# Retention and two MLPs on one core: the key-value product of a head pair as two 64x64 products on the diagonal

## The reference

```python
state = np.zeros((B, H, D, D))                 # B=4, H=8, S=768, D=64
for t in range(S):
    state = gamma[None, :, None, None] * state + np.einsum('bhd,bhe->bhde', k[:, :, t], v[:, :, t])
    y[:, :, t] = scale * np.einsum('bhd,bhde->bhe', q[:, :, t], state)
```

## Time and profile before

| | before |
|---|---|
| median of 3 runs | 1049.16 us (1048.57 to 1049.89) |
| span of the profiled execution | 1048.8 us |
| TensorE matmul busy | 1023.9 us (98%) |
| VectorE busy | 460.4 us (44%) |
| ScalarE busy | 431.9 us (41%) |
| GpSimd busy | 90.4 us (9%) |
| mean granted TensorE clock | 0.995 |

### The profile page before, as it was taken

One profiled execution on the slowest core, in us unless ns is written; L12 is line 12 of the kernel. 1 busy time (PEld: TensorE's weight loads), 2 busy tenths in 40 slices (PEclk: granted clock), 3 DMA queues, 4 the chain that ended last, 5 costly groups with the idle time before them and its releaser, 6 DMA issues.

```text
span 1048.8 us, 15480 instructions
## 1 busy us (share of the span) xinstructions
PE 1023.9 (98%) x5496; PEld 900.6 (86%) x5496; DVE 460.4 (44%) x874; ACT 431.9 (41%) x776; POOL 90.4 (9%) x101
## 2 busy tenths in 40 slices
PE   6799999999998999999999999999999999999998
PEld 4489999999998999999999888888888888888886
DVE  3847635356352463433324653253253254244243
ACT  3445333243231442413223464364364264265255
POOL 5321110111001011100000000000000000000000
PEclk9999999999999999999999999999999999999999
DMA  7664331532314234313134403013012012012000
GB/s 229 210 217 146 106 108 52 166 114 93 119 46 138 98 113 136 111 51 120 66 115 135 137 21 101 1 60 100 0 60 90 10 60 90 10 60 91 11 21 31
DMA packets 75656, 95.51 MB, mean 91 GB/s; under 512 B 7248, under 2 KB 59728, under 8 KB 75600
## 3 DMA queue, kind: packets, MB, share of 16 engines
q1 hardware_dynamic: 71856, 81.11, 24.1%
q0 software_dynamic: 3744, 13.63, 3.9%
HBM read 64.04 MB, written 30.67 MB: 90 GB/s over the span
## 4 chain that ended last, share of the span: by engine, by line
PE 93%; DVE 2%; DMA 1%; ACT 1%; issue 1%; SPq 0%; POOL 0%; DVEq 0%; ACTq 0%; POOLq 0%
PE psum L284 28%; PE psum L286 28%; PE psum L285 27%; PE psum L521 3%; PE psum L531 3%; PE psum L609 2%; PE psum L513 1%; DMA w_raw<-weights 1%; PE psum L548 1%; DMA v_buf<-v_rows 0%; PE psum L501 0%; DVE w_gv_lo L936 0%; ACT L802 0%; DMA chunk_decay_t<-chunk_decay 0%; DVE probs L897 0%
## 5 line engine op out<-in xcount | busy, mean ns | idle before, releaser
L284 PE MATMUL psum<-xn_hi,w_gv_hi 128*128 128x384 f32 x768 | 267.1, 348 | 1.0 <-issue 1.0
L286 PE MATMUL psum<-xn_hi,w_gv_lo 128*128 128x384 f32 x768 | 258.4, 336 | 2.6 <-issue 2.6
L285 PE MATMUL psum<-xn_lo,w_gv_hi 128*128 128x384 f32 x768 | 257.7, 336 | 0.0
L764 ACT ACTIVATE silu<-psum 128x384 f32<-128x384 f32 x96 | 47.2, 492 | 283.6 <-PE psum L286 283.6
L284 PEld LDWEIGHTS psum<-xn_hi,w_gv_hi 128*128 128x128 f32 x768 | 145.2, 189 | 4.3 <-issue 3.4
L286 PEld LDWEIGHTS psum<-xn_hi,w_gv_lo 128*128 128x128 f32 x768 | 144.9, 189 | 2.9 <-issue 2.9
L285 PEld LDWEIGHTS psum<-xn_lo,w_gv_hi 128*128 128x128 f32 x768 | 145.3, 189 | 0.9
L998 DVE TENSOR_TENSOR act_buf<-psum,silu 128x384 f32<-128x384 f32 x96 | 53.5, 557 | 199.9 <-PE psum L286 116.7
L284 PE MATMUL psum<-act_hi,w_out_hi 128*128 128x512 f32 x288 | 114.2, 397 | 0.0
L286 PE MATMUL psum<-act_hi,w_out_lo 128*128 128x512 f32 x288 | 112.3, 390 | 0.0
L285 PE MATMUL psum<-act_lo,w_out_hi 128*128 128x512 f32 x288 | 112.3, 390 | 0.0
(11 more groups left out here) (82 smaller groups left out, 1453.2 us busy)
## 6 DMA issues: line engine op xcount, KB each, us to landing
act_dram<-act_buf SPq DMA_DIRECT2D x96, 192.0 KB, 1.8
act_raw<-act_dram SPq DMA_DIRECT2D x72, 256.0 KB, 2.8
w_raw<-weights POOLq DMA_DIRECT2D x26, 512.0 KB, 4.9
kq_buf<-k_t SPq DMA_DIRECT2D x32, 192.0 KB, 2.8
kq_buf<-q_t SPq DMA_DIRECT2D x64, 96.0 KB, 2.9
k_buf<-k_rows SPq DMA_DIRECT2D x32, 192.0 KB, 2.9
v_buf<-v_rows SPq DMA_DIRECT2D x32, 192.0 KB, 3.1
out<-out_buf SPq DMA_DIRECT2D x24, 256.0 KB, 2.0
```

The lines of the kernel that those rows point to most:

```text
L284: pe.matmul(dst, w_hi, m_hi, start=start, stop=False)
L285: pe.matmul(dst, w_hi, m_lo, start=False, stop=False)
L286: return pe.matmul(dst, w_lo, m_hi, start=False, stop=stop)
L764: act.activation(silu[:, f % 2, :], psum[:, GATE[f % 2], 0:TB], ACT.Silu).then_inc(silu_ready, 1)
```

## The change

The product of decayed keys and values is made as two products, one for each head: 64 stationary columns (the head's decayed keys) against 64 moving columns (the head's values), written to the block on the diagonal that belongs to the head. The two blocks off the diagonal aren't computed any more; nobody read them. The semaphore is incremented by the second product. Nothing else changes.

```diff
                 at_least(pe, state_ready, 2 * (b * BKV + states_before(ch)))
-                pe.matmul(psum[:, KV, 0:P], k_dec[:, r % 2, i, :],
-                          v_buf[:, q, i * P:(i + 1) * P], start=True, stop=True).then_inc(kv_done, 1)
+                for h in range(2):
+                    span = slice(h * HD, (h + 1) * HD)
+                    mm = pe.matmul(psum[span, KV, span], k_dec[:, r % 2, i, span],
+                                   v_buf[:, q, i * P + h * HD:i * P + (h + 1) * HD], start=True, stop=True)
+                mm.then_inc(kv_done, 1)
```

## The result

| | before | after |
|---|---|---|
| median of 5 runs | 1048.57 us (1047.48 to 1049.89) | 1041.79 us (1037.13 to 1042.33) |
| ratio | | 0.9913, 95% interval 0.9888 to 0.9939 |
| span of the profiled execution | 1048.8 us | 1040.0 us |

What follows compares the result with a forecast made beforehand. TensorE, busy 1023.9 of 1048.8 us, was taken as the bound. 1048.8 - 7.0 (products) - 0.4 (half clock) + 0.1 (slack) = 1041.5 us of span, plus 0.36 to the median: 1041.9 us, range 1039.5 to 1046.0.

Steps and rivals of the forecast that it cites:

- Product before, 0.22 us: Retention steps on TensorE: the old two-pass product delays the outputs by 0.22 us, 0.43 with it against 0.21 without.
- The charge for the change of form: TensorE switching from 128*128 to 128*64 matmuls: about 0.09 us, moved ahead of the product and still paid once.
- Two heads side by side, a pass of 0.055, load and stream overlapped: New product on TensorE: two passes delay the outputs by 0.11 us, saving 0.11 to 0.12, taken as 0.115.
- 61 products on the path, slack of 0.1: Of 80 products, 61 at full clock save 0.115 us each, 7.0 in all; VectorE's split keys take back 0.1.
- The product at 74.6 us: Not on the path: TensorE waits 0.6 us for VectorE's split keys behind it, so shortening it only lengthens a wait.
- 0.4 us at half clock in the start: Two products on the path, at 20.5 and 49.3 us, save 0.2 us each at half clock.
- What the program's length may do: 320 more executed instructions may change the gaps and clock at the loop's jump; counted as no change, 1.7 us either way.
- the two gaps: TensorE's waits called issue, 1.0 and 2.6 us, where the loop starts over at 323 us; half clock follows for 3.4 us.
- Rival 1: New passes run one behind the other or load and stream don't overlap: 0.22 us as now, 1049 us; chance 0.09.
- rival 2: TensorE can't be fed the eight instructions per product, limiting from 0.055 us per matmul: up to 1058 us; chance 0.06.
- rival 3: Steps get shorter but waits for VectorE take back 19 of 61 products' gain: 5.1 us saved, 1044 us; chance 0.05.
- its milder estimate of 1.6 us: At about 62 ns of sequencer per matmul a product costs 248 ns: kernel some 1.6 us slower, 1050.8 us.

Runs made afterwards that it cites:

- twice_b: Changed kernel with each pair of narrow products made twice; one execution 1044.3 us, 0.608 us from last scores to the outputs' second pair.
- one_half: Changed kernel with both narrow products on the same half of the array's columns, second head's outputs wrong; median 1042.4 us, ratio 0.9906.
- pad_before: Kernel before the change with 40 more do-nothing semaphore instructions between the gate matmuls of batch 0; 1047.26 against 1051.87 us, ratio 0.995.
- rest_only: Kernel before the change, given the narrow products in batches 1 to 3 only, old product in batch 0; median 1039.44 us, ratio 0.9876.

## Why the prediction was right, and where it was wrong

- **Product before, 0.22 us, read from steps with and without it.** Right: doubling it costs 0.223.
- **The charge for the change of form moves and isn't paid twice.** Right: 0.21 from scores to the new matmuls, none between these and the outputs.
- **Two heads side by side, a pass of 0.055, load and stream overlapped.** Right: 0.107 saved per step (forecast 0.11 to 0.12), and 0.01 more in the gate matmuls behind it, which I hadn't foreseen; on one half of the array it is lost, with twice the width it is lost, doubled it costs 0.116.
- **61 products on the path, slack of 0.1.** About right in sum: 60 products behind 65 us gave 6.9 us; 61 x 0.115 was 7.0. Measured from the gate matmul ahead of a step to the one behind it, 55 of the 60 steps are 0.10 to 0.11 us shorter. The product at 74.6 us is hidden as I said: TensorE's next wait for the split keys is longer by what it saved. TensorE's scores matmul behind it, before and after:

```profile
78.23 0.36 PE L284 MATMUL psum<-kq_hi 128*128 128x256 f32 x1 [0.57 <-DVE kq_lo L904]
80.55 0.35 PE L284 MATMUL psum<-kq_hi 128*128 128x256 f32 x1 [0.68 <-DVE kq_lo L907]
```

  The slack runs out at 120 us (0.09 lost) and at 253 and 391 us (0.03 each), 0.15 where I took off 0.1, and at 85.7 us, which I had missed (0.13).
- **0.4 us at half clock in the start.** Not resolved: the start varies by 6 us with the clock.
- **What the program's length may do.** This is the step that failed. I saw the two gaps and the half clock behind them, wrote that they may shrink, counted no change, and allowed 1.7 us for the clock alone. The term that I put at nothing measured 4.35 us: 2.6 of gap and 1.7 of clock. The change's 160 instructions ahead of the loop moved its head from 6 instructions before the end of a piece to 102. The gap's place, two matmuls behind the head, and the count of added instructions were both at hand, and such a gap, which needs the head in the last 40 or so of 256 instructions, is likelier to go than to stay when the code moves.
- **Rivals.** Rival 1 is refuted by the steps, rival 2 by twice_b (0.035 us a matmul; its milder estimate of 1.6 us should read 61 x 0.028 = 1.7), rival 3 by the stretches (from 65 us to the head they gave 4.5 us for 40 products).
- **The time.** 1041.9 met 1041.79 by luck: in the profiled executions the head's 4.35 us stood against a slow start of 1.9 + 0.4, so a product term that was right met two omissions of opposite sign. With the start as before, the first trace would have ended at about 1037.7 us of span.

## What to carry to other kernels

Before counting an edit that changes the number of instructions ahead of a loop, look at the gaps called issue behind the loop's jump. If one follows the first within a few instructions, the head may lie at the end of a code piece, and then most insertions, useful or not, take the gap away (40, 80, 160, 208 and 480 instructions did here; 256 brought it back); a padding of do-nothing instructions tests that at once. Two 64-column products on different halves of TensorE's columns cost as one here, and where a neighbour already uses that form, the change of form is paid anyway. Compare kernels by stretches between matmuls that both share: a total with an interval of 5 us would have given one_half, which saves nothing in a step, the same verdict as the change.

## What the runs showed of the hardware

- A change between the 128*128 and the 128*64 form adds about 0.09 us over the pace (0.21 from scores to the first narrow matmul against 0.12), in every trace.
- Products on different column halves don't keep program order between them by their start times: in one_half an output matmul started at 206.63 us, ahead of a pass at 206.69 that stands earlier in the program, and so at 76 of 80 products. Whether the end times follow the program's order, these records, whose ends are modelled, can't show.
- Eight narrow float32 matmuls with their loads went through in 0.28 us. The Trainium skill ("TensorE: Matmul & The Clock Gate", section "Wait — 56ns, not 53.3ns?") has about 62 ns of the sequencer per MATMUL with hardware decoding off, as an estimate 0.50 us for the eight; the trace disagrees for this burst. Which way of decoding was on, and whether a long run of such matmuls would be held up, no run here shows.
- A loop's jump can cost twice: 1.0 us for the piece of code with the head, and 2.5 to 2.6 us more, with 3.4 to 6.8 us of half clock behind it, where the head lies 6 instructions ahead of the end of its piece. With 38 or more there was no second gap.
- The same code up to the first gate matmul (old product) took 47.2 us at full clock in pad_before and 53.4 us at a mean of 0.86 in rest_only.
